# Running a second mixture-of-experts layer inside the search that assigns its tokens

## The reference

```
logits = x @ w_gate
flat = logits.flatten()
order = np.argsort(-flat)
assigned = -np.ones(N); counts = np.zeros(E)
for idx in order:
    tok, e = idx // E, idx % E
    if assigned[tok] >= 0 or counts[e] >= cap: continue      # cap = N // E = 384
    assigned[tok] = e
    counts[e] += 1
for e in range(E):                                          # 8 experts
    mask = assigned == e
    out[mask] = np.maximum(x[mask] @ w1[e], 0.0) @ w2[e]    # 512 -> 1024 -> 512
```

## Time and profile before

| | us |
|---|---|
| three runs | 1203.68, 1199.72, 1204.15 (median 1203.68) |
| profiled execution: device time / span of its instructions | 1199.88 / 1198.1 |
| TensorE busy | 925.9 (77%) |
| VectorE busy | 569.3 (48%) |
| ScalarE busy | 324.3 (27%) |
| GpSimd busy | 228.3 (19%) |

### The profile page before, as it was taken

The page is one execution under the profiler, slowest core; times in us unless marked ns, Lnnn a source line. Parts: engine busy times, 40 slices in busy tenths (PEclk is TensorE's granted clock), DMA queues, the critical chain, the costliest instruction groups (busy, mean ns, idle before and its releaser), DMA issues.

```text
span 1198.1 us, 23541 instructions
## 1 busy us (share of the span) xinstructions
PE 925.9 (77%) x7460; PEld 761.5 (64%) x7461; DVE 569.3 (48%) x1602; ACT 324.3 (27%) x659; POOL 228.3 (19%) x339
## 2 busy tenths in 40 slices
PE   5999999258999999999943332222269999999995
PEld 4787787246888888888832222222158888888883
DVE  5766657663222222222236677777734444445431
ACT  2555445052222222222230000000023443434420
POOL 5643332011111211112110000000012222222220
PEclk9999999569999999999975555555579999999998
DMA  9668673444111111111111000000023543445300
GB/s 186 132 129 169 122 150 67 154 167 168 36 35 35 44 44 35 35 35 35 44 27 67 0 0 0 0 0 0 0 97 115 185 164 125 147 152 184 114 30 24
DMA packets 45988, 97.48 MB, mean 81 GB/s; under 512 B 7248, under 2 KB 19584, under 8 KB 45952
## 3 DMA queue, kind: packets, MB, share of 16 engines
q1 hardware_dynamic: 27200, 59.55, 17.2%
q0 software_dynamic: 8064, 26.46, 6.7%
q10 hardware_dynamic: 10688, 11.01, 4.6%
HBM read 77.49 MB, written 19.51 MB: 81 GB/s over the span
## 4 chain that ended last, share of the span: by engine, by line
PE 62%; issue 26%; DVE 6%; POOL 2%; DMA 2%; ACT 1%; DVEq 0%; ACTq 0%; SPq 0%; POOLq 0%
PE bank L688 43%; PE bank L600 3%; PE bank L712 3%; PE bank L581 3%; PE bank L641 2%; PE bank L695 2%; PE bank L735 2%; PE bank L618 2%; PE bank L590 1%; DMA q_eye<-in_q 1%; PE bank L728 1%; PE bank L632 1%; DVE ksum L1016 1%; ACT W L896 1%; DVE W L1210 1%
## 5 line engine op out<-in xcount | busy, mean ns | idle before, releaser
L688 PE MATMUL bank<-W,xh 128*128 (+1 forms) x784 | 253.8, 405 | 13.4 <-DVE gates L1216 10.6
L688 PE MATMUL bank<-W,hh 128*128 (+1 forms) x784 | 253.0, 404 | 11.6 <-DVE hl L1223 11.6
L688 PEld LDWEIGHTS bank<-W,xh 128*128 128x128 f32 x784 | 145.7, 191 | 45.9 <-issue 11.2
L688 PEld LDWEIGHTS bank<-W,hh 128*128 128x128 f32 x784 | 145.8, 191 | 44.0 <-issue 10.3
L688 PE MATMUL bank<-W,hl 128*128 (+1 forms) x392 | 156.4, 399 | 0.0
L688 PE MATMUL bank<-W,xl 128*128 (+1 forms) x392 | 155.9, 398 | 0.0
L779 PE MATMUL bank<-ge,cb 128*8 128x16 bf16 x1344 | 42.3, 172 | 106.6 <-DVE ge L1335 106.6
L1223 DVE TENSOR_TENSOR hl<-bank,hh 128x512 fp32r<-128x512 f32 x98 | 63.1, 686 | 96.9 <-ACT hh L896 91.5
L779 PEld LDWEIGHTS bank<-ge,cb 128*8 128x8 bf16 x1344 | 36.1, 83 | 111.9 <-DVE ge L1335 111.9
L896 ACT ACTIVATE xh<-bank 128x512 fp32r<-128x512 f32 x50 | 29.8, 595 | 268.5 <-PE bank L695 268.5
L520 POOL COPY sidx<-idx 128x1 int32 (+1 forms) x49 | 27.3, 556 | 368.4 <-DVE y L1231 249.2
(11 more groups left out here) (238 smaller groups left out, 1322.8 us busy)
## 6 DMA issues: line engine op xcount, KB each, us to landing
raw_w<-in_moe_w SPq DMA_DIRECT2D x20, 2048.0 KB, 9.4
va<-in_v_win SPq DMA_DIRECT2D x16, 585.0 KB, 6.3
k_raw<-in_k SPq DMA_DIRECT2D x16, 384.0 KB, 9.4
q_eye<-in_q ACTq DMA_DIRECT2D x16, 384.0 KB, 7.2
x_rows<-x ACTq DMA_DIRECT2D x12, 384.0 KB, 9.1
x_rows<-x SPq DMA_DIRECT2D x4, 387.0 KB, 7.2
xg<-x_rows,gidx POOLq DMA_INDIRECT x26, 3.4
y_rows<-y,sidx POOLq DMA_INDIRECT x25
```

Source lines behind the costliest of these rows:

```text
L688: last = mm(ps, lhs[a][:, c, :], rhs[b](c), start=c == 0 and t == 0, stop=c == n - 1 and t == 2)
```

## The change

The second layer's experts are no longer computed after the search but inside it. There are now 10 phases, `for ph in range(E + 2)`, written out instead of looped. In phase ph the search (ph < 7) shuts an expert; the expert shut one phase earlier (r = ph - 1) is prepared: its tokens are ranked and listed, its rows gathered, turned and split, its weights split; and the expert shut two phases earlier (q = ph - 2) is computed. `build_slots(1)`, the hidden rows' transposes and the old `step2` are gone.

- **TensorE** cuts an expert's products into 28 segments of 6 matmuls: 16 of `hidden` (now with the weight stationary and all 384 rows moving, so that the hidden rows come out already turned: 96 matmuls of 384 columns), then 12 of `outward` (72 matmuls of 512 columns). Three segments stand in each search step: one between the count and the spread, two between the spread and the next count; the last four stand between the phase's closing pieces. `rank_mine` stands in step 1, `list_mine` in step 5, and a `turn_rows` (four transposes) after segments 19, 23 and 27.
- **VectorE** keeps the search and gets, in its order, the hidden rows' low parts (8), `mark_mine` (step 0), `place_mine` (step 1), `take_list` (step 5), the gathered rows' low parts (3), and at the end of the phase the four low parts of the second weight.
- **GpSimd** makes the one-hots by which the tokens are listed (`picks`: 24 pairs of instructions, each waiting for the one before it, and two more), gathers the three tiles, and makes the four low parts of the first weight (`low_parts`). It stores the outputs last.
- **ScalarE** does the ReLU and high part in one pass (`hidden_high`), the high parts of weights and rows, and the output copies.
- **SyncE** loads expert r's weights when its number is known (`eid_ready`), straight to where the low parts will stand. The first layer's guessed weights are loaded a little earlier.

```diff
-            with pe.Fori(0, E - 1) as ph:
-                for t in range(STEPS):
-                    ... (24 counts, one spread)
-            build_slots(1)
-            step2(...)                      # 24 tiles
+            def hidden(q, fc, half):
+                if fc == 0 and half == 0:
+                    pe.wait_ge(xlow_done, GT * (q + 1))
+                    pe.wait_ge(low_done, W1U * (q + 1))
...
+                for c in range(KC // 2 * half, KC // 2 * half + KC // 2):
+                    for t, (w, a) in enumerate(((w1h, xh2), (w1h, xl2), (w1l, xh2))):
+                        last = mm(bank[fc % 2][:, 0:CAP], w[:, q % 2, c, f], a[:, c, :], ...)
+                for t in range(STEPS):
+                    if ph < PH:
+                        count(ph, t)
+                    segment(3 * t)
+                    if t == RANKS_AT and 0 <= r < E:
+                        rank_mine(r)
+                    if ph < PH:
+                        any_full(ph, t)
+                    segment(3 * t + 1)
+                    if t == LIST_AT and 0 <= r < E:
+                        list_mine(r)
+                    segment(3 * t + 2)
...
+            def picks(r):                                            # GpSimd
+                pool.wait_ge(places_ready, r + 1)
+                for j in range(TC):
+                    chain2(g.tensor_scalar(slot_hot[:, j, :], iota_l[:, :], mlo[:, j:j + 1], mine[:, j:j + 1], ALU.is_equal, ALU.mult))
+                    chain2(g.tensor_scalar(mtile[:, j, :], iota_t[:, 0:GT], mhi[:, j:j + 1], None, ALU.is_equal))
+                chain2(g.tensor_tensor(msel[:, :, 0, :], mtile[:, :, :], ..., ALU.mult))
+                chain2(g.tensor_tensor(msel[:, :, 1, :], mtile[:, :, :], ..., ALU.mult))
+            def low_parts(r):                                        # GpSimd
+                for u in range(W1U):
+                    pool.wait_ge(high_done, (W1U + W2U) * r + u + 1)
+                    g.tensor_tensor(low, whole, high.bitcast(F32), ALU.subtract).then_inc(low_done, 1)
+            for ph in range(E + 2):
+                q, r = ph - 2, ph - 1
+                if 0 <= r < E:
+                    picks(r)
+                    for t in range(GT):
+                        gather_second(r, t)
+                    low_parts(r)
+                if q >= 0:
+                    for t in range(GT):
+                        store_second(q, t)
...
+            def place_mine(r):                                       # VectorE
+                dve.wait_ge(ranked, r + 1)
+                ... (nine short instructions on 128x24)
+                vec.tensor_copy(mhi[:, :], mposi[:, 2, :]).then_inc(places_ready, 1)
+                if ph < PH:
+                    find(ph)
+                if 0 <= r < E:
+                    rows_low(r, 1)
+                if ph < PH:
+                    choose(ph)
+                    shut(ph)
+                if 0 <= r < E:
+                    for u in range(2):
+                        weight_low(r, u)
+                    rows_low(r, 2)
+                    for u in range(2, W2U):
+                        weight_low(r, u)
```

More of the change, by code:

```diff
@@ new lines, in two_layers_of_experts @@
+        ix = sc("ix", [P, TC])
+        cf = sc("cf", [P, TC, E])
+        cb = sc("cb", [P, TC, E], BF16)
+        free = sc("free", [P, TC])
+        open8 = sc("open8", [P, E])
+        shut8 = sc("shut8", [P, E])
+        room = sc("room", [E, 1])
+        rtmp8 = sc("rtmp8", [E, 4])
+        known = sc("known", [P, 1], I32)
+        sign = sc("sign", [P, 1], I32)
+        digit = sc("digit", [P, 1], I32)
+        top = sc("top", [P, 1])
+        weights = sc("weights", [P, KSEARCH], I32)
+        thr0 = sc("thr0", [P, KSEARCH], I32)
@@ L146, in two_layers_of_experts @@
+        rem = sc("rem", [P, 1])
+        tied = sc("tied", [P, TC], BF16)
+        tk = sc("tk", [P, TC])
+        tkb = sc("tkb", [P, TC], BF16)
+        ttot = sc("ttot", [P, TC])
+        tinc = sc("tinc", [P, TC])
+        second.close()
+        below = sb("below", [P, 68 * 256])
         const_ready = sem("const_ready")
@@ L254, in two_layers_of_experts @@
[L254 to L265, removed]
@@ L546, in _ @@
             base = base + 2 * tiles - 4
[L547 to L558, removed]
@@ L564, in _ @@
+            for t in range(GT):
+                pool.wait_ge(out_stored[t], 16 * E)
         @block.tensor
@@ new lines, in outward @@
+            def outward(q, t, part):
+                if part == 0:
+                    if t == 0:
+                        pe.wait_ge(w2_low_done, W2U * (q + 1))
+                    if GT * q + t >= 2:
+                        pe.wait_ge(out_copied, GT * q + t - 1)
+                if t == 0:
+                    pe.wait_ge(hlow_done, FC * q + 2 * part + 2)
+                rows = slice(P * t, P * t + P)
+                for c in range(2 * part, 2 * part + 2):
+                    for n, (a, w) in enumerate(((hh2, w2h), (hh2, w2l), (hl2, w2h))):
+                        last = mm(bank[2 + t % 2][:, :], a[:, c, rows], w[:, q % 2, c, :], start=c == 0 and n == 0, stop=c == FC - 1 and n == 2)
+                if part == 3:
+                    last.then_inc(out_done, 1)
@@ L1289, in _ @@
             chain.start(base)
-            for u in range(W1U):
-                split_lo(1, u, 0, 0)
+            chain = Chain(dve, dve_chain2)
             chain(vec.memset(free[:, :], 1.0))
```

496 lines of the change are left out of this document (323 added, 173 removed).

## The result

The changed kernel took 1311.26 us (median of 4 runs, 1309.8 to 1312.5) against 1202.25 for the kernel before: a ratio of 1.091 (95% interval 1.088 to 1.094), 9% slower. The forecast was 1182, and 1311 lies outside its range of 1120 to 1240.

What follows compares the result with a forecast made beforehand. Bound: a search chain between VectorE and TensorE, then TensorE alone. Phases 32.3 + 60 + 324.2 + 87.2 + 33.6 and tail 13.1 make 550.4 us against 569.2, 18.8 less: forecast 1182 us, range 1120 to 1240.

Steps and rivals of the forecast that it cites:

- GpSimd, the unknown: Double phases, picks before the list: 0.61 us a pair, 15 us undisturbed, taken at 21; wait 4 us (bounds 0 and 14).
- rival B: GpSimd sets the pace: the list waits for picks every phase; 0.1 us more per instruction gives 1236 us; chance 0.20.
- The room at the list: From `place_mine`'s end, TensorE has about 17 us of steps 2 to 5 before it comes to the list.
- The forecast's waits: Waits at the list: 4 us per double phase, 8 in phase 1, 3.3 in phases 7 and 8 each.
- The mutual hold: Beside the search, GpSimd and VectorE each wait for the other's whole instruction; picks taken at 21 us instead of 15.
- the two pairs of rows: Profile: VectorE's 0.22 us instruction took 0.76 beside a GpSimd copy; GpSimd's 0.19 us copy took 1.01 beside VectorE subtractions.
- TensorE's own work, its waits and its clock: Double phase: 43.6 us of products and search matmuls, 11.7 waiting for VectorE, 2.6 for low clock after a gap.
- The gap at the phase's end: End of a double phase: VectorE needs 10.3 us, TensorE has 2.5 us of work and waits 7.8 us.
- Phase 0, phase 9 and the tail: Phase 0, search only, 32.3 us; phase 9, 33.6 us; tail from last output copy to end, 13.1 us.
- GpSimd's low parts: Four GpSimd subtractions of 1024 elements per phase, 2.2 us each, holding VectorE; taken at 4 us per double phase.
- Rival C: TensorE's clock stays low in double phases: some 30 us more in five phases, 1332 us; chance 0.02.
- rival D: A missed wait puts expert work in series with the search: 76 us instead of 65.9 in five phases, 1232; chance 0.06.

## Why the prediction was wrong

- **The step that failed is "GpSimd, the unknown": the price of a pair**, put at 0.61 us from a cast and a one-column copy, with an upper bound of 0.5 us for either instruction. It measured 0.80 + 0.31 us with two gaps, 1.30. The bound was no bound: it was near twice a cast, and nothing in the trace of before showed this kind of instruction. By itself it takes three times the cast of the same size. The mechanism of rival B was right, and so was its place; each instruction cost 0.35 us more than the sum had it, where B tried 0.1.
- **The room at the list** (about 17 us) was near: picks of 33.0 us less 14.4 of waiting leave 18.6. The forecast's waits summed to 5 x 4 + 8 + 2 x 3.3 = 35 us; they measured 130.5. That is 96 of the 129 us missed. Moving the low parts of the first weight off GpSimd gave back 24. The clock goes with the gaps: it was 0.81 in a double phase of the changed kernel, in which TensorE was busy 53.7 us, against 0.87 and 52.1 with the one-hots on VectorE. How much of the rest is the clock alone was not separated.
- **The mutual hold.** I let it stretch the picks from 15 to 21 us. It stretched them by 1 us (32.0 us undisturbed in phase 7, 33.0 beside a search), and the pairs without waits hardly held VectorE either. So the wait behind each is not what lets VectorE in; why these instructions do and the subtractions do not is open. For the low parts I had 4 us a phase; from the kernel with whole to the one with cut low parts a double phase went from 68.5 to 59.5, so 9.0, because I let each subtraction hold VectorE for itself, and one instruction was held through all four. The Trainium skill (SBUF — State Buffer, section "SBUF: two separate sides") has the pair locked for one whole instruction; the 9.09 us row shows more than that. Of the two pairs of rows that I set beside it, only the second has a VectorE instruction with two inputs; the first is a TENSOR_SCALAR with one tensor.
- **TensorE's own work, its waits and its clock** (43.6 + 11.7 + 2.6 = 57.9 us) were right as a sum: 59.5 us in the mean without either of GpSimd's costs. The terms were less so: TensorE was busy in 49.9 of these, where 43.6 + 2.6 stood, and idle in 9.6, where 11.7 stood. The two errors partly cancel. The gap at the phase's end was 7.09 us where 7.8 stood. Phase 0, phase 9 and the tail were within 1 us.
- **GpSimd's low parts**: 2.37 us where 2.2 stood.
- **Rival C** (low clock) and **rival D** (no overlap) are out: with the cut low parts a double phase is 59.5 us at a clock of 0.93, where C had some 96 and D 76.

That the version with the one-hots on VectorE lands on the forecast's 1182 is partly luck: it has no wait at the list, and over twice the hold I had given it.

## What to carry to other kernels

Before work goes to GpSimd, get that very form of instruction timed, by itself, at its size; multiply by their number and compare with the room the waiting engine has, since a neighbour of another kind may be off by three times, and an upper bound taken from such a neighbour is none. Where GpSimd has several two-input instructions next to each other beside a VectorE that is on the path, look in the trace for small VectorE instructions as long as the whole run of them, and try cutting the run or a wait between its members: here it was worth 27 to 45 us, but not every piece size helped. An overlapped schedule should be judged by its phases against TensorE's own sum; here that sum was good to 2 us, partly by errors that cancel, and pointed to each of the three costs left (the wait at the list, the hold, the gap at the phase's end).

## What the hardware showed that I had not expected

- GpSimd's compare-and-multiply with two scalars: 0.80 us for 128 columns, 0.57 for 64; with one scalar and one operation 0.60 for 128 columns and 0.31 for three; a cast of 128 columns 0.26.
- A VectorE instruction of 0.17 us was held for 9.09 us by four GpSimd subtractions in a row, 9.6 by eight, 13.0 by 32, and 0.6 by the first of 16. With a gap of 0.18 us between the four, it was held 2.5 us. A run of 48 of GpSimd's TENSOR_SCALAR instructions without waits held it for 0.40 us at most.
- After TensorE had stood still for 6.8 us, its granted clock was 0.50 in the 2.9 us from 829.00 on. The hold cost 9.0 us a phase in place of 6.8; that the clock is the difference is an inference.
